# Attention and two feed-forward blocks on one core: where the reciprocals of the softmax sums are written out and spread on SyncE's DMA queue

## The chip, the core and the metric

The kernel runs on one core of one Trainium2 chip. The metric is the device time of one execution in microseconds (us). Before the change it was 748.28 us, the median of 3 runs (746.96 to 752.52).

## The reference

Sixteen heads (2 batches of 8) of 768 tokens and width 64 go through a clustered attention, and the result through two feed-forward blocks. A query sees only the keys whose nearest centroid is its own.

```python
q_assign = np.argmax(np.einsum('bhsd,hcd->bhsc', q_n, c_n), axis=-1)
k_assign = np.argmax(np.einsum('bhsd,hcd->bhsc', k_n, c_n), axis=-1)
mask = q_assign[:, :, :, None] == k_assign[:, :, None, :]
scores = scale * np.matmul(q, k.transpose(0, 1, 3, 2))
scores = np.where(mask, scores, -1000000000.0)
attn = np.exp(scores - max); attn = attn / (sum(attn) + 1e-09)
x = attn @ v                      # then, as (1536 tokens, 512):
x = ((x @ w1) * (x @ w2) @ w3) @ w_out      # as written: h = a * b @ w3
out = (h * clip(h + 3, 0, 6) / 6) @ moe2_w_out,  h = x @ moe2_w_in
```

## The kernel before

The program has three stretches. Up to about 66 us weights are folded (w_out with w3) and the first heads are made ready. From there to about 300 us it does the attention, and after that the two feed-forward blocks with 7-product and 3-product schemes on pieces of 128 x 384. The change touches the attention alone.

**Slots and units.** A slot is one tile of 128 queries of one head against all 768 keys; there are 96 (`SLOTS`). Two heads make a pair of 12 slots, and the slots of a pair are ordered so that 3 tiles of the even head come first, then 3 of the odd head (unit 2p), and then the other 3 and 3 (unit 2p+1). A unit is 6 slots; there are 16. So even head n is first used in slot 6n and odd head n in slot 6n-3.

**One slot.** TensorE makes the scores of slot s+2 (`score`, L1338 and L1340) into one of two PSUM tiles, and can do so only when the exponentials of slot s have left it. VectorE takes the row maximum (`row_max`, L1057), ScalarE the exponential with its row sums (L750). TensorE then transposes the probabilities (L1350), ScalarE and VectorE copy them to `probs_t` (L839, L1117), and TensorE multiplies by V a unit later (`p_times_v`, L1364). Once in a unit TensorE also computes the cluster logits of a coming head (L1308), their columns (L1317) and the one-hot rows (L1325). In iteration s of its loop TensorE issues the scores of slot s+2 first. All engines run through the same iterations, each in its own order.

**The sums.** In the iteration that opens unit u+1 (s = 6u+6) VectorE does, in this order: the row maximum of slot s+2, the reciprocals of unit u's sums (`reciprocals(u)`, L1062 and L1064, which raises the semaphore `s_recip`), and then `x_normed(u-1)` (L1070), which multiplies the attention output of the unit before by its reciprocals. That needs the reciprocals spread over the partitions in `recip_all`. The row maximum of the next slot stands behind it.

**The spreading** goes over DRAM, on SP's queue. `spread_recips(u)` (from L486) waits for `s_recip`, writes the 768 reciprocals to `recip_rows` (L489), waits until they have landed (`s_rrow`), and reads them back twice with a broadcast into `recip_all` (L493, two DMAs, `s_rall`).

**SP's queue.** SP issues its DMAs in the order of the program text, and a wait stops all that follows. For each head n from 2 on:

- `load_ops(n)` (L453): 4 DMAs that copy the split operands of head n to one of three `qk_ops` buffers. It waits until the scores of the head that had the buffer, n-3, are all made: slot 6n-10 for odd n, 6n-13 for even n.
- `load_raw(n+2)` (L465): one DMA, q and k of a later head from DRAM.
- `load_mask(n)` (L459): 6 DMAs that copy the one-hot rows under the operands, after ScalarE has copied them out of PSUM (L742).
- `load_v` (L470): 2 DMAs, for odd n from 5 on.
- `spread_recips(n-3)` for n from 3 on.

The last three units are spread behind the loop, and then the weight blocks of the feed-forward stretch follow on the same queue (L421).

Of the kernel before, what the change touches and what calls it, by code (L numbers as in the profile page):

```python
# [16 lines left out]
ST = S // P  # L17
# [32 lines left out]
def last_slot(n):  # L50

    return n // 2 * 2 * ST + ST + n % 2 * 3 + 2
# [24 lines left out]
def ring_bank(use):  # L77
    return RING[use] % len(RING_BANKS)


def ring_turn(use):

    return RING[use] // len(RING_BANKS)
# [129 lines left out]
def program(nc: bass.Bass, qk, v, cent, wo, w3, w12, wio, out):  # L213
    with ExitStack() as ctx:
        def sem(name):
            return ctx.enter_context(nc.semaphore(name))
# [4 lines left out]
        def sb(name, shape, dt=F32, at=None):  # L221
            size = 4
            for n in shape[1:]:
                size *= n
            size += -size % 64
            if at is None:
                at, top[0] = top[0], top[0] + size
            assert at + size <= nc.sbuf_usable_end, (name, at + size)
            return nc.alloc_sbuf_tensor_at(name, shape, dt, offset=at)
# [23 lines left out]
        sums1, recips = sb("sums1", [P, SLOTS]), sb("recips", [P, SLOTS])  # L253
# [51 lines left out]
        recip_rows = nc.dram_tensor("recip_rows", (2, 2 * HALF), F32, kind="Internal").ap()  # L305
# [18 lines left out]
        s_recip, s_rrow, s_rall = sem("recips_ready"), sem("recip_rows_in"), [sem(f"recips_spread{i}") for i in range(2)]  # L324
# [28 lines left out]
        def x_cols(unit):  # L353

            b, tile = divmod(unit // 2, KT)
            at = tile * TOK + b * S + unit % 2 * HALF
            return slice(at, at + HALF)
# [40 lines left out]
        def _(sp):  # L398
# [42 lines left out]
            def load_ops(n):  # L441
                sp.wait_ge(s_split, 2 * n + 2)
                if n == 2:
                    sp.wait_ge(s_up, F1T)
                if n >= 3:
                    sp.wait_ge(s_scores, last_slot(n - 3) + 1)
                ops, split, done = qk_ops[n % 3], qk_split[n % 2], s_opq[n % 3]
                q_hi = split[0:D, 0:1, :].to_broadcast([D, 2, S])
                for first, operands, source in (
                    (0, slice(0, 2), q_hi), (D, slice(0, 1), split[0:D, 1:2, :]),  # L450
                    (0, slice(2, 4), split[D:P, :, :]), (D, slice(2, 3), split[D:P, 0:1, :]),
                ):
                    sp.dma_start(ops[first:first + D, operands, :].bitcast(F32), source.bitcast(F32)).then_inc(done, 16)  # L453

            def load_mask(n):
                sp.wait_ge(s_rel[ring_bank(("hot", n))], ring_turn(("hot", n)) + 1)
                for rows in range(ST):
                    t = rows % SPANS * 2 + rows // SPANS
                    sp.dma_start(qk_ops[n % 3][D:MASK_ROWS, 1:4:2, t * P:(t + 1) * P].bitcast(F32),  # L459
                                 hot_rows[n % 2][rows * C:(rows + 1) * C, :, :].bitcast(F32)).then_inc(s_opm[n % 3], 16)  # L460

            def load_raw(n):
                sp.wait_ge(s_split, 2 * n - 2)
                sp.wait_ge(s_fill[ring_bank(("logits", n - 2))], ring_turn(("logits", n - 2)) + 1)
                sp.dma_start(qk_raw[n % 2][:], qk[n]).then_inc(s_raw[n % 2], 16)  # L465

            def load_v(n):
                if n >= 4:
                    sp.wait_ge(s_pv, n // 2 * 2 - 2)
                sp.dma_start(v_raw[n % 4][:].rearrange("p t d -> p (t d)"), v[n]).then_inc(s_v[n % 4], 16)  # L470
# [12 lines left out]
            load_mask(1)  # L483
            for n in range(4):
                load_v(n)
            def spread_recips(u):  # L486
                sp.wait_ge(s_recip, u + 1)
                rows = recip_rows[u % 2]
                sp.dma_start(rows.rearrange("(k p t) -> p k t", k=2, t=3),  # L489
                             recips[:, u * ST:(u + 1) * ST].rearrange("p (k t) -> p k t", k=2)).then_inc(s_rrow, 16)  # L490
                sp.wait_ge(s_rrow, 16 * (u + 1))
                for k in range(2):
                    sp.dma_start(recip_all[k * D:(k + 1) * D, x_cols(u)], rows[k * HALF:(k + 1) * HALF].partition_broadcast(D)  # L493
                                 ).then_inc(s_rall[u % 2], 16)

            for n in range(2, HEADS):
                load_ops(n)
                if n + 2 < HEADS:
                    load_raw(n + 2)
                load_mask(n)  # L500
                if n % 2 == 1 and n >= 5:
                    load_v(n - 1)
                    load_v(n)
                if n >= 3:
                    spread_recips(n - 3)
            for u in range(UNITS - 3, UNITS):
                spread_recips(u)
            for n in range(GATE0 + 2, BLOCKS):
                load_next(n)
# [1086 lines left out]
```

## Time and profile before

| | us |
|---|---|
| median of 3 runs | 748.28 (746.96 to 752.52) |
| the profiled execution | 747.12 |
| its span, first to last instruction | 745.1 |

| engine | busy us | share of the span |
|---|---|---|
| PE (TensorE matmuls) | 713.6 | 96% |
| DVE (VectorE) | 470.3 | 63% |
| ACT (ScalarE) | 415.7 | 56% |
| POOL (GpSimd) | 444.3 | 60% |

The profile is one execution, recorded by the hardware. PE is busy nearly all the time, so the question for any change is in which stretches it is not, and what it waits for there. The mean TensorE clock granted over the span is 0.995 of full speed. SPq is the DMA-issuing instructions of SyncE: they are not counted as busy time, but the timeline shows how long each takes. In the chain of work that ended last, TensorE has 68%, DMA 9% and SP's queue 8% of the span.

### The profile page before, as it was taken

To read this page: it belongs to the slowest core of one execution; us is meant where nothing else is said; L and a number is where in the kernel's file an instruction comes from. 1 tells how busy PE (TensorE), PEld (TensorE's weight loads), DVE (VectorE), ACT (ScalarE), POOL (GpSimd) and SP (SyncE) were. 2 spreads that over 40 slices of the span, in tenths; PEclk is the share of its full clock that TensorE was granted. 3 is DMA by queue.
4 is the path that set the end of the run, shared out by engine and by line. 5 is a ranking of instruction groups with operands and counts; after the bars stand their busy time and mean duration, and the time that the engine had idled before them with its cause. 6 is when DMAs were issued, how large, how long until landed. Compare 5 with 4: busy or idle time off the path is not lost.

```text
span 745.1 us, 11781 instructions
## 1 busy us (share of the span) xinstructions
PE 713.6 (96%) x4001; PEld 599.5 (80%) x4001; DVE 470.3 (63%) x706; ACT 415.7 (56%) x855; POOL 444.3 (60%) x453
## 2 busy tenths in 40 slices
PE   6998999988999899999999999999999999999998
PEld 4776666655666466799999999999998779998886
DVE  5326666755666567477886778878865435885221
ACT  6225667656666578444455454467754446775333
POOL 4963343434434356599696996968647748762321
PEclk9999999999999999999999999999999999999999
DMA  9555655555555440121000220002211223221212
GB/s 317 151 150 137 145 144 125 137 122 152 135 124 123 102 100 12 68 86 57 29 29 29 85 70 17 29 29 86 79 63 58 70 81 132 73 72 58 70 43 84
DMA packets 41482, 68.48 MB, mean 92 GB/s; under 512 B 10192, under 2 KB 17360, under 8 KB 41424
## 3 DMA queue, kind: packets, MB, share of 16 engines
q1 hardware_dynamic: 39840, 64.85, 30.6%
q10 hardware_dynamic: 1584, 2.88, 1.0%
q8 instruction: 32, 0.52, 0.3%
q14 instruction: 26, 0.21, 0.1%
HBM read 44.07 MB, written 3.19 MB: 63 GB/s over the span
## 4 chain that ended last, share of the span: by engine, by line
PE 68%; DMA 9%; SPq 8%; DVE 5%; ACT 4%; issue 2%; POOL 2%; ACTq 0%; DVEq 0%; POOLq 0%
PE ps L1260 19%; PE ps L1261 19%; PE ps L1262 18%; SPq L459 5%; DMA recip_rows<-recips 4%; PE ps L1364 3%; DMA recip_all<-recip_rows 3%; PE ps L1350 3%; PE ps L1338 3%; PE ps L1340 2%; DMA stage<-in_w 2%; SPq L453 1%; DVE g_lo L1176 1%; ACT probs L750 1%; DVE sum_lo L1078 1%
## 5 line engine op out<-in xcount | busy, mean ns | idle before, releaser
L596 POOL TENSOR_TENSOR b_lo<-stage,b_hi 128x512 fp32r<-128x512 f32 x94 | 111.7, 1190 | 109.8 <-ACT b_hi L822 107.9
L1176 DVE TENSOR_TENSOR g_lo<-gate,g_hi 128x384 fp32r<-128x384 f32 x96 | 79.7, 838 | 69.1 <-ACT g_hi L882 68.9
L1057 DVE TENSOR_REDUCE neg_max<-ps 128x1 f32<-128x768 f32 x96 | 91.5, 953 | 48.8 <-PE ps L1340 48.8
L882 ACT CAST g_hi<-gate 128x384 fp32r<-128x384 f32 x96 | 48.8, 514 | 83.8 <-PE ps L1262 83.7
L750 ACT ACTIVATE probs<-ps,neg_max 128x768 f32<-128x768 f32 x96 | 86.7, 904 | 15.0 <-DVE neg_max L1057 13.4
L1350 PE MATMUL ps<-ident,probs 128*128 128x128 f32 x576 | 79.9, 275 | 0.6 <-ACT probs_t L839 0.6
L1260 PE MATMUL ps<-b_hi,g_hi 128*128 128x512 f32 x192 | 75.0, 390 | 2.1 <-DVE g_lo L1176 2.1
L1364 PE MATMUL ps<-probs_t,v_raw 128*64 128x384 f32 x384 | 76.3, 507 | 0.0
L839 ACT COPY probs_t<-ps 128x512 f32<-128x512 f32 x96 | 54.4, 585 | 38.5 <-PE ps L1350 38.3
L1261 PE MATMUL ps<-b_lo,g_hi 128*128 128x512 f32 x192 | 74.8, 390 | 0.0
L1262 PE MATMUL ps<-b_hi,g_lo 128*128 128x512 f32 x192 | 74.8, 390 | 0.0
L1078 DVE TENSOR_TENSOR sum_lo<-sum_raw,sum_hi 128x768 fp32r<-128x768 f32 x64 | 64.3, 1009 | 14.7 <-ACT sum_hi L798 14.4
L1350 PEld LDWEIGHTS ps<-ident,probs 128*128 128x128 f32 x576 | 67.3, 141 | 5.9 <-ACT probs_t L839 1.1
L1338 PE MATMUL ps<-qk_ops 128*128 128x512 f32 x192 | 58.5, 386 | 13.3 <-ACT probs L750 11.8
L1151 DVE TENSOR_TENSOR part<-part,ps 128x384 f32<-128x384 f32 x96 | 51.7, 548 | 26.8 <-PE ps L1262 23.2
L798 ACT CAST sum_hi<-sum_raw 128x768 fp32r<-128x768 f32 x64 | 39.4, 617 | 48.8 <-POOL sum_raw L611 30.9
L554 POOL TENSOR_TENSOR hot_cols<-hot,best 128x192 f32<-128x192 f32 x16 | 8.2, 513 | 85.4 <-DVE best L1053 85.4
L859 ACT COPY part<-ps 128x384 f32<-128x384 f32 x96 | 45.9, 478 | 21.7 <-PE ps L1262 21.4
L1338 PEld LDWEIGHTS ps<-qk_ops 128*128 128x128 f32 x192 | 29.2, 191 | 33.6 <-ACT probs L750 21.0
L822 ACT CAST b_hi<-stage 128x512 fp32r<-128x512 f32 x94 | 51.7, 550 | 1.9 <-ACT out_sb L902 1.9
L1340 PE MATMUL ps<-qk_ops 80*128 80x512 f32 x192 | 49.8, 340 | 0.0
L562 POOL TENSOR_TENSOR x_lo<-x_raw,x_hi 128x384 fp32r<-128x384 f32 x15 | 15.0, 1000 | 55.8 <-ACT x_hi L755 55.8
(119 smaller groups left out, 1871.3 us busy)
## 6 DMA issues: line engine op xcount, KB each, us to landing
stage<-in_wio SPq DMA_DIRECT2D x64, 256.0 KB, 2.5
stage<-in_w SPq DMA_DIRECT2D x48, 256.0 KB, 3.1
qk_ops<-qk_split SPq DMA_DIRECT2D x32, 384.0 KB, 5.1
qk_raw<-in_qk SPq DMA_DIRECT2D x16, 384.0 KB, 5.4
qk_ops<-qk_split SPq DMA_DIRECT2D x32, 192.0 KB, 4.8
v_raw<-in_v SPq DMA_DIRECT2D x16, 192.0 KB, 2.6
recip_all<-recip_rows SPq DMA_DIRECT2D x32, 96.0 KB, 2.9
out<-out_sb ACTq DMA_DIRECT2D x11, 256.0 KB, 2.1
```

The source lines that it names most:

```text
L596: nc.gpsimd.tensor_tensor(b_lo[n % 2][:, cols], stage[n % 2][:, cols], b_hi[n % 2][:, cols].bitcast(F32), ALU.subtract).then_inc(s_lo[half ...
L750: nc.scalar.activation(probs[g % PROBS][:], scores[g % 2], ACT.Exp, bias=neg_max[:, g:g + 1], scale=1.0, accum_out=sums[:, g:g + 1]).then_ ...
L1057: nc.vector.tensor_reduce(neg_max[:, g:g + 1], scores[g % 2], AX.X, ALU.max, negate=True).then_inc(s_max, 1)
L1078: nc.vector.tensor_tensor(sum_lo[g % 2][:, cols], sum_raw[:, cols], sum_hi[g % 2][:, cols].bitcast(F32), ALU.subtract).then_inc(s_sum_lo, 1)
L1176: nc.vector.tensor_tensor(g_lo[i][:], hidden(q, c, f)[0][:], g_hi[i][:].bitcast(F32), ALU.subtract).then_inc(s_glo, 1)
L1260: nc.tensor.matmul(psum, w_hi, m_hi, start=start, stop=False, skip_group_check=read_between)
L1261: nc.tensor.matmul(psum, w_hi, m_lo, start=False, stop=False, skip_group_check=read_between)
L1262: return nc.tensor.matmul(psum, w_lo, m_hi, start=False, stop=stop, skip_group_check=read_between)
L1338: nc.tensor.matmul(tile[:, cols], ops[:, 0, q], ops[:, 2, cols], start=True, stop=False)
L1340: mm = nc.tensor.matmul(tile[:, cols], ops[0:MASK_ROWS, 1, q], ops[0:MASK_ROWS, 3, cols], start=False, stop=True)
L1350: mm = nc.tensor.transpose(bank[:, c * P:(c + 1) * P], probs[s % PROBS][:, (j - ST * i) * P:(j - ST * i + 1) * P], ident[:])
L1364: mm = nc.tensor.matmul(ps[side * D:(side + 1) * D, PV_BANKS[unit % 2], 0:HALF].rearrange("p (a b) -> p a b", a=3), v_raw[(unit // 2 * 2 + ...
```

## The change

`spread_recips` is divided in two. `store_recips(u)` waits for the reciprocals and writes them out; it now stands directly behind `load_ops`, ahead of `load_raw` and `load_mask`. `spread_recips(u)` waits until they have landed and reads them back; it now stands behind `load_mask`, and ahead of the two `load_v`. Behind the loop, for the last three units, the two parts follow each other as before. No transfer is added or left out, and no other engine's program differs.

```diff
-            def spread_recips(u):
-                sp.wait_ge(s_recip, u + 1)
-                rows = recip_rows[u % 2]
-                sp.dma_start(rows.rearrange("(k p t) -> p k t", k=2, t=3),
-                             recips[:, u * ST:(u + 1) * ST].rearrange("p (k t) -> p k t", k=2)).then_inc(s_rrow, 16)
-                sp.wait_ge(s_rrow, 16 * (u + 1))
+            def store_recips(u):
+                sp.wait_ge(s_recip, u + 1)
+                sp.dma_start(recip_rows[u % 2].rearrange("(k p t) -> p k t", k=2, t=3),
+                             recips[:, u * ST:(u + 1) * ST].rearrange("p (k t) -> p k t", k=2)).then_inc(s_rrow, 16)
+
+            def spread_recips(u):
+                sp.wait_ge(s_rrow, 16 * (u + 1))
+                rows = recip_rows[u % 2]
                 for k in range(2):
                     sp.dma_start(recip_all[...], rows[...].partition_broadcast(D)).then_inc(s_rall[u % 2], 16)

             for n in range(2, HEADS):
                 load_ops(n)
+                if n >= 3:
+                    store_recips(n - 3)
                 if n + 2 < HEADS:
                     load_raw(n + 2)
                 load_mask(n)
+                if n >= 3:
+                    spread_recips(n - 3)
                 if n % 2 == 1 and n >= 5:
                     load_v(n - 1)
                     load_v(n)
-                if n >= 3:
-                    spread_recips(n - 3)
             for u in range(UNITS - 3, UNITS):
+                store_recips(u)
                 spread_recips(u)
```

On SP's queue, for an odd head (n = 5, whose one-hot rows are in `hot_rows_74`), from the last operand copy on; rows with - stand there before the change, rows with + after it:

```order
 L453 DMA qk_ops_59<-qk_split_63 64x768
+L488 DMA recip_rows<-recips 128x2x3 [waits recips_ready]
 L465 DMA qk_raw_61<-in_qk 128x768 [waits ring_filled0,qk_split]
 L459 DMA qk_ops_59<-hot_rows_74 16x2x128 [waits ring_released0]
 L459 DMA qk_ops_59<-hot_rows_74 16x2x128 x5
+L495 DMA recip_all<-recip_rows 64x384 [waits recip_rows_in]
+L495 DMA recip_all<-recip_rows 64x384
 L470 DMA v_raw_69<-in_v 128x384 [waits pv_filled]
 L470 DMA v_raw_70<-in_v 128x384 [waits pv_filled]
-L489 DMA recip_rows<-recips 128x2x3 [waits recips_ready]
-L493 DMA recip_all<-recip_rows 64x384 [waits recip_rows_in]
-L493 DMA recip_all<-recip_rows 64x384
```

The writing-out has moved ahead of 7 DMAs and, like the spreading, ahead of the two loads of V, which now come last.

On SP's queue, for the even head before it (n = 4), up to the first operand copy of head 5:

```order
 L453 DMA qk_ops_58<-qk_split_62 64x768
+L488 DMA recip_rows<-recips 128x2x3 [waits recips_ready]
 L465 DMA qk_raw_60<-in_qk 128x768 [waits ring_filled0,qk_split]
 L459 DMA qk_ops_58<-hot_rows_73 16x2x128 [waits ring_released0]
 L459 DMA qk_ops_58<-hot_rows_73 16x2x128 x5
-L489 DMA recip_rows<-recips 128x2x3 [waits recips_ready]
-L493 DMA recip_all<-recip_rows 64x384 [waits recip_rows_in]
-L493 DMA recip_all<-recip_rows 64x384
+L495 DMA recip_all<-recip_rows 64x384 [waits recip_rows_in]
+L495 DMA recip_all<-recip_rows 64x384
 L453 DMA qk_ops_59<-qk_split_63 64x2x768 [waits scores_filled,qk_split]
```

Only the writing-out has moved; the wait for the reciprocals (`recips_ready`) now stands ahead of the raw load and the one-hot rows.

## Rows read from the trace of the kernel before

**Rows 1.** Windows by start and end: length, busy time, PE clock, DMA share.

```profile
core 0: us, PE busy (x) PEld busy (x) DVE busy (x) ACT busy (x) POOL busy (x), PEclk, DMA share, GB/s
124.19:138.50 14.31, 14.31 (x96) 9.58 (x95) 9.76 (x17) 10.06 (x22) 6.44 (x9) 1.00 0.60 129
138.50:156.53 18.03, 15.87 (x97) 10.71 (x95) 9.99 (x17) 10.57 (x23) 7.45 (x10) 0.91 0.58 150
247.00:251.40 4.40, 4.40 (x21) 2.00 (x21) 1.65 (x2) 2.41 (x5) 3.71 (x5) 0.63 0.55 139
309.00:745.00 436.00, 428.99 (x2282) 403.01 (x2281) 287.28 (x391) 230.00 (x476) 298.94 (x277) 1.00 0.18 62
```

**Rows 2.** Waits of PE, 60 to 310 us: total us, times, longest.

```profile
PE ps L1338 <- ACT probs L750: 11.8, 9, 3.5
```

**Rows 3.** Timeline of PE: start, length, instruction, idle before and its releaser.

```profile
79.20 0.63 PE L1308 MATMUL ps<-qk_raw,cent_t 128*32 128x256 f32 x6
...
131.09 0.52 PE L1340 MATMUL ps<-qk_ops 80*128 80x512 f32 x2
...
148.11 0.61 PE L1338 MATMUL ps<-qk_ops 128*128 128x512 f32 x2
...
152.68 1.01 PE L1338 MATMUL ps<-qk_ops 128*128 128x512 f32 x2 [2.16 <-ACT probs L750]
...
250.37 1.08 PE L1308 MATMUL ps<-qk_raw,cent_t 128*32 128x256 f32 x6
```

**Rows 4.** Timeline of DVE around two turns of the reciprocals.

```profile
133.59 0.19 DVE L1064 RECIPROCAL recips<-sums 128x6 f32<-128x6 f32 x1
...
147.89 0.19 DVE L1064 RECIPROCAL recips<-sums 128x6 f32<-128x6 f32 x1
150.53 0.66 DVE L1070 TENSOR_TENSOR x_raw<-ps,recip_all 128x384 f32<-128x384 f32 x1 [2.44 <-DMA recip_all<-recip_rows]
```

**Rows 5.** Waits of DVE, 66 to 278 us: total us, times, longest.

```profile
DVE x_raw L1070 <- DMA recip_all<-recip_rows: 14.1, 9, 3.8
```

**Rows 6.** Timeline of SP's queue for head 7: start, length, DMAs.

```profile
131.68 3.79 SPq L453 DMA_DIRECT2D qk_ops<-qk_split  x4
135.57 1.75 SPq L465 DMA_DIRECT2D qk_raw<-in_qk  x1
137.36 4.48 SPq L459 DMA_DIRECT2D qk_ops<-hot_rows  x6
141.88 1.05 SPq L470 DMA_DIRECT2D v_raw<-in_v  x2
142.98 0.43 SPq L489 DMA_DIRECT2D recip_rows<-recips  x1
145.80 1.13 SPq L493 DMA_DIRECT2D recip_all<-recip_rows  x2
```

**Rows 7.** Chain of work that ended last, pieces from 140 to 158 us.

```profile
146.34 4.10 DMA recip_all<-recip_rows
...
151.64 0.99 ACT probs L750 x2
```

**Rows 8.** Waits of SP's queue, 66 to 273 us.

```profile
SPq L493 <- DMA recip_rows<-recips: 36.7, 13, 5.5
SPq L446 <- PE ps L1340: 8.7, 5, 2.9
```

**Rows 9.** Line 489, all 16 writings-out: from issue to landing.

```profile
DMA to landing us min/median/max: 2.2/3.1/5.9
```

**Rows 10.** Line 493, all 32 spreadings: from issue to landing.

```profile
DMA to landing us min/median/max: 2.5/2.9/4.1
```

**Rows 11.** Line 453, operand copies: from issue to landing.

```profile
DMA to landing us min/median/max: 3.8/4.7/6.1
```

**Rows 12.** Line 459, one-hot rows: from issue to landing.

```profile
DMA to landing us min/median/max: 1.8/2.3/4.1
```

## The prediction

> **What bounds the kernel now.** I read the windows first, then the waits of TensorE, then the chain of work back from one such wait, and last the timeline of SP's queue against VectorE's. After 309 us the change moves nothing, and TensorE is busy 428.99 of 436.00 us there [rows 1]; all that can be won or lost lies in the attention. There TensorE has a pace of its own. From one set of logits to the next is one unit, and the unit from 124.19 to 138.50 us has no idle time: 14.31 us at full clock. The next one takes 18.03 us with 15.87 busy, at a mean clock of 0.91 [rows 1]. Between the logits at 79.20 and those at 250.37 us lie 11 units in 171.17 us [rows 3]; at 14.31 each they would take 157.41, so 13.8 us are lost there. The waits of TensorE say to whom: nine times, 11.8 us in all, the scores (L1338) wait for an exponential [rows 2].
>
> What holds the exponential is seen in the unit of 138.50 to 156.53. VectorE ends the reciprocals of a unit at 148.08 (147.89 + 0.19) and could do x_normed then; it starts it at 150.53, having waited 2.44 us for the spread reciprocals [rows 4]. The row maximum queued behind it is late, so are the two exponentials at 151.64 [rows 7], and the scores at 152.68 come after 2.16 us idle [rows 3]. So the wait on VectorE costs TensorE all but 0.3 us. VectorE has nine such waits, 14.1 us [rows 5]; less 0.3 each that is 11.4, and TensorE's nine are 11.8 [rows 2]: the same ones. And SP is what makes the reciprocals late: it stands 36.7 us in 13 waits between writing out and spreading, and for scores, its wait when it is ahead of TensorE, only 5 times, 8.7 us [rows 8].
>
> **What the change does to an odd head.** Head 7 is a clean case, since SP is on time for it. Its trigger is the end of the scores at 131.61 (131.09 + 0.52) [rows 3], and the copies start at 131.68 [rows 6]. VectorE's turn at 148.08 [rows 4] is 16.5 us behind the trigger: one unit of 14.31 plus 2.2. Before, the spreading lands at 150.44 (146.34 + 4.10) [rows 7], 18.8 us behind the trigger, so 2.4 late even with SP on time. After the change, by the same rows [rows 6]:
>
> - spreading starts at 145.80. Taken away: the loads of V ahead of it (142.98 - 141.88 = 1.10) and all from the start of the writing-out to the spreading (145.80 - 142.98 = 2.82). Added ahead: the issue of the writing-out, up to 0.6 us with its gap (0.43 here; I take the larger). So 142.5.
> - if it lands as slowly as it did here (0.54 to the second issue, then 4.10), that is 147.1, 1.0 us before the turn. With the median 2.9 [rows 10] it is 145.9, 2.1 us before.
>
> So the wait goes to nothing with a slack of 1.0 to 2.1 us. The bounds of that landing are the 2.5 and 4.1 of the same transfers [rows 10]; it now follows the one-hot rows directly, and I take 3.5, nearer to the upper end, because nothing drains the queue ahead of it any more. The slack is then 1.5 us.
>
> **The writing-out now lies behind the operand copies.** It is issued 3.9 us after the first of them, and the spreading asks for it at 142.5, about 6.9 us behind its issue (135.6). Before it took 2.2 to 5.9 us to land [rows 9]. The cost of its new place is not in the trace. Lower bound: as before, 3.1, wholly hidden under the raw load and the six one-hot issues (1.75 + 4.48 us [rows 6]). Upper bound: it can only start to count when the last copy, issued about 1 us earlier, has landed, up to 6.1 us after its issue [rows 11], and then takes its worst 5.9: 5.1 + 5.9 = 11.0 us, 4.1 too late. With the medians it is 3.7 + 3.1 = 6.8 us, which just fits. I take 0 for it, as it fits and 1.5 us of slack stand behind; the upper bound makes a rival below.
>
> The Trainium skill (DMA: Bandwidth & Descriptors, section "Queues, rings and completion order") speaks against the change here. It says that descriptors are consumed in ring order, and that the increment of the semaphore is a strongly ordered write, which lands only after that engine's earlier writes. By it the 3 KB would wait for some 1.1 MB of copies ahead of them, so the 3.7 us would always be paid and the landing would be at least 3.7 + 2.2 = 5.9 us. No row here shows a small transfer directly behind these copies, so it is open whether the trace agrees; even by the rule the sum stays as it is, since 5.9 and 6.8 both lie within the 6.9.
>
> **The wait for the reciprocals now stands ahead of raw load and one-hot rows.** For an odd head the reciprocals of unit n-3 are ready at 133.78 (133.59 + 0.19) [rows 4], 2.2 us behind the trigger, and the copies keep SP until 135.5 [rows 6]: no wait. For the even head 8 behind it: SP starts its copies when head 7 is done, 142.5 + 1.13 + 1.10 + gaps = 144.8, and has issued them at 148.7; the reciprocals are ready at 148.08: no wait. Then writing-out, raw load and one-hot rows (0.6 + 1.8 + 4.0) and the spreading (1.2 to issue) take it to 156.3, and the spreading lands at 158.6 to 159.9. The turn is at 148.08 + 14.31 = 162.4. The next trigger, 2 x 14.31 behind the last one, is at 160.2, so SP has 3.9 us to spare in each pair and comes on time to the next odd head. Before, the same sum is longer by two waits of 2.2 us or more each (2.82 less the issue), so SP has nothing to spare: that is why heads further on are late by more than 2.4 us (up to 3.8 [rows 5]).
>
> **The other moves.** The one-hot rows of head 7 are issued 0.6 us later, the last at 141.9, landing by 144.2 to 146.0 [rows 12]. TensorE's first scores of head 7 are those at 148.11 [rows 3]: at least 2.1 us of cover. The loads of V move behind the spreading by 1.2 us; they are for products two units on. Both cost nothing. For the last three units the order is as before.
>
> **The sum.** Idle time: 11.8 us [rows 2]. Half clock: after the two longest waits TensorE is granted less for a while. The unit of 18.03 us has 3.72 more than 14.31, of which 2.16 idle, so 1.56 from the clock; the stretch from 247.00 lasts 4.40 us at a mean of 0.63 [rows 1], 4.40 x 0.37 = 1.6. Together 15.0 us. Against the units: 13.8 for the eleven, and the rest falls behind 250.37. I keep back 0.6 us for a few landings at the upper end: 14.4 us. Of the profiled execution's 747.1 us that leaves 732.7; the median of the runs is 1.2 us higher and gives 733.9. I forecast 733.5 us.
>
> **The rivals.**
> - The writing-out lands late (**rival A**, 0.12). If the last copy must land and HBM be slow as well, the spreading waits up to 4.1 us. Beyond 1.5 us of slack and TensorE's 0.3 it costs 2.3 us in each of the seven odd heads (3 to 15) whose turns were late: 16 us, nothing is left of the gain. In the middle, with landings of 9.9 us (3.0 late), it is 1.2 x 7 = 8 us, so 741 us. For it: nothing shows the new place. Against: the medians fit.
> - Another wait takes the place (**rival B**, 0.07). A unit after a stalled one may run at 14.31 us only because the stall gave the others time. Then the pace would be that of SP or VectorE, and the time 744 to 749 us. Against: in the clean unit VectorE is busy 9.76 and ScalarE 10.06 of 14.31 us, and GpSimd 6.44 [rows 1]; SP's issues sum to some 12 us of 14.31.
> - The one-hot rows of the odd heads come late (**rival C**, slower, 0.03). They now follow one more transfer and land among a queue that never drains. It decides from a landing of 6.2 us (148.11 - 141.9), against 4.1 at most now [rows 12]. To be slower by 1% they would have to cost 15.0 + 7.5 us over seven heads, 3.2 us each beyond that point, landing after 9.4 us: 756 us.
>
> **How the numbers follow.** My forecast, a gain of 12 to 15.5 us, has 0.78; the rivals have 0.12, 0.07 and 0.03. More than 1% (7.5 us) is what a measurement can tell from none. Faster: 0.78 and half of A, 0.84. Same: the rest of A and B, 0.13. Slower: C, 0.03. Lower end of the range: the fastest run, 746.96, less 15.0, less 1.5 for what the runs scatter: 730.5. Upper end: the middle of A, 741.
>
> **What would show it.** Right: no wait for the spread reciprocals on VectorE ahead of L1070 before the last units, and TensorE's 11.8 us of L1338 waiting for L750 gone; 14.3 us from logits to logits in all units; SP waiting for scores ahead of every odd head's copies, several us each. Wrong: SP still waiting for the written-out rows ahead of the spreading by more than 1.5 us in odd heads (A), VectorE still waiting in x_normed, or TensorE waiting for a DMA of `qk_ops` (C). It would also be wrong if the units ran at 14.31 us and the feed-forward stretch grew in return.

## The result, and the profile of the changed kernel

| | before | changed |
|---|---|---|
| median of 4 runs, us | 749.94 (746.96 to 752.52) | 731.43 (730.17 to 731.85) |
| the profiled execution, us | 747.12 | 731.85 |
| its span, us | 745.1 | 729.8 |
| mean TensorE clock over the span | 0.995 | 1.000 |

The ratio of the runs is 0.9752, with a 95% interval of 0.9708 to 0.9796: 18.5 us faster. Between the two profiled executions it is 15.3 us, because that of the kernel before was one of its faster ones.

The first view is the page's list of the chain that ended last, by engine. Before it had DMA and SP's queue with 17% together.

```profile
PE 89%; DVE 5%; ACT 3%; POOL 2%; issue 1%; DMA 1%; ACTq 0%; SPq 0%; POOLq 0%
```

DMA now has 1% and SP's queue none. The windows and the timeline of TensorE show the attention. (The lines of this kernel are 5 higher than before from `spread_recips` on: L1313 was L1308, L1330 was L1325, L1343 was L1338, L1345 was L1340, L1069 was L1064, L1075 was L1070. L488 writes out and L495 spreads.)

```profile
77.64:234.94 157.30, 157.30 (x1037) 105.39 (x1035) 107.24 (x177) 110.50 (x232) 66.57 (x87) 1.00 0.74 145
```

```profile
77.64 0.63 PE L1313 MATMUL ps<-qk_raw,cent_t 128*32 128x256 f32 x6
...
144.27 0.42 PE L1330 MATMUL ps<-ident,hot_cols 128*96 128x128 f32 x2
144.44 0.60 PE L1343 MATMUL ps<-qk_ops 128*128 128x512 f32 x2
...
234.94 0.63 PE L1313 MATMUL ps<-qk_raw,cent_t 128*32 128x256 f32 x6
```

The same eleven units that took 171.17 us in [rows 3] take 157.30 us, and TensorE is busy in all of them: 14.30 us each, the pace of the one clean unit of [rows 1]. The group of [rows 2] is gone from its waits. What is left between 60 and 295 us is small, and stood there before too (its two longest items are shown):

```profile
PE ps L1330 <- POOL hot_cols L563: 2.2, 2, 1.4
PE ps L1355 <- ACT probs_t L844: 0.6, 2, 0.3
```

The waits of SP's queue between 66 and 262 us answer to [rows 8]:

```profile
SPq L446 <- PE ps L1345: 25.4, 7, 4.2
SPq L488 <- DVE recips L1069: 3.2, 1, 3.2
SPq L495 <- DMA recip_rows<-recips: 1.9, 1, 1.9
```

The 36.7 us in 13 waits for written-out rows are now 1.9 us in one, and that one and the 3.2 us for the reciprocals are behind the loop, where nothing was moved. In their place SP waits 25.4 us in 7 times for TensorE's scores, 3.6 us ahead of each odd head: it is no longer what is late. Head 7 again, on SP's queue and on VectorE, as in [rows 4, 6]:

```profile
128.02 3.75 SPq L453 DMA_DIRECT2D qk_ops<-qk_split  x4
131.81 1.80 SPq L488 DMA_DIRECT2D recip_rows<-recips  x1
133.71 0.71 SPq L465 DMA_DIRECT2D qk_raw<-in_qk  x1
134.46 4.34 SPq L459 DMA_DIRECT2D qk_ops<-hot_rows  x6
138.85 1.23 SPq L495 DMA_DIRECT2D recip_all<-recip_rows  x2
140.13 1.06 SPq L470 DMA_DIRECT2D v_raw<-in_v  x2
```

```profile
144.23 0.19 DVE L1069 RECIPROCAL recips<-sums 128x6 f32<-128x6 f32 x1
144.38 0.67 DVE L1075 TENSOR_TENSOR x_raw<-ps,recip_all 128x384 f32<-128x384 f32 x1
```

The spreading starts 10.8 us behind the first copy (138.85 - 128.02), where it was 14.1 (145.80 - 131.68). With 0.64 us to the second of the two and the median landing of 3.0 it has landed at 142.5 (in this head it took 2.7, so 142.2); VectorE's turn comes at 144.4 and it goes straight on. The slack by the median is 1.9 us. By their own landings it is 1.4 to 2.3 us over the seven odd heads, 2.2 in head 7.

**Where 15.3 us of the span went.** The attention from the first of those logits to the first product of the feed-forward stretch took 221.5 us and now takes 206.0: 15.4 us less. The rest is two differences that cancel. The stretch ahead of it was 1.6 us shorter and the feed-forward stretch 1.7 us longer (444.4 against 446.1 us). Both are taken up with the experiments.

### The profile page after: what moved, and what is told of

The parts are those of the page before. It is cut to its first block, busy times and chain, and to the rows that moved or that the text cites. A ratio compares the mean times of both kernels' runs of the same rounds, so it can differ in the third digit from the quotient of the medians.

```text
span 729.8 us, 11781 instructions
## 1 busy us (share of the span) xinstructions
PE 711.2 (97%) x4001; PEld 598.6 (82%) x4001; DVE 468.1 (64%) x706; ACT 415.8 (57%) x855; POOL 442.1 (61%) x453
## 4 chain that ended last, share of the span: by engine, by line
PE 89%; DVE 5%; ACT 3%; POOL 2%; issue 1%; DMA 1%; ACTq 0%; SPq 0%; POOLq 0%
PE ps L1265 20%; PE ps L1266 19%; PE ps L1267 19%; PE ps L1369 10%; PE ps L1355 8%; PE ps L1343 5%; PE ps L1345 4%; DVE g_lo L1181 2%; PE ps L1313 1%; DVE sum_lo L1083 1%; PE ps L1330 1%; DMA stage<-in_w 1%; PE ps L1322 1%; ACT out_sb L907 1%; POOL b_lo L601 1%
## 5 line engine op out<-in xcount | busy, mean ns | idle before, releaser
L1083 DVE TENSOR_TENSOR sum_lo<-sum_raw,sum_hi 128x768 fp32r<-128x768 f32 x64 | 64.3, 1008 | 14.4 <-ACT sum_hi L803 14.1
L1343 PE MATMUL ps<-qk_ops 128*128 128x512 f32 x192 | 58.2, 384 | 0.0
L1345 PE MATMUL ps<-qk_ops 80*128 80x512 f32 x192 | 49.5, 339 | 0.0
L1175 DVE SCALAR_TENSOR_TENSOR gate<-gate,part 128x384 f32<-128x384 f32 x48 | 38.5, 801 | 15.1 <-ACT gate L873 15.1
L873 ACT ACTIVATE gate<-part,three 128x384 f32<-128x384 f32 x48 | 29.8, 620 | 27.7 <-DVE part L1156 27.7
```

What stands on the lines that cost most here:

```text
L1083: nc.vector.tensor_tensor(sum_lo[g % 2][:, cols], sum_raw[:, cols], sum_hi[g % 2][:, cols].bitcast(F32), ALU.subtract).then_inc(s_sum_lo, 1)
L1343: nc.tensor.matmul(tile[:, cols], ops[:, 0, q], ops[:, 2, cols], start=True, stop=False)
L1345: mm = nc.tensor.matmul(tile[:, cols], ops[0:MASK_ROWS, 1, q], ops[0:MASK_ROWS, 3, cols], start=False, stop=True)
```

## The experiments

All are compared with the kernel before on the same chip. In the four comparisons its medians were 749.9, 744.1, 748.9 and 748.5 us. The changed kernel was run in the first and, as a control, in the last of them, at 731.4 and 732.2 us; the other kernels are set against these two times, some of them from another comparison.

| experiment | median us | ratio to before, 95% |
|---|---|---|
| no reciprocals over DRAM | 730.76 | 0.9796 to 0.9855 |
| divided in odd heads only | 731.06 | 0.9797 to 0.9854 |
| divided in even heads only | 746.30 | 0.9973 to 1.0040 |
| divided, V ahead of the spreading | 731.23 | 0.9803 to 0.9868 |
| in one piece, ahead of V | 743.88 | 0.9907 to 0.9962 |
| spreading directly behind writing-out | 742.85 | 0.9889 to 0.9952 |
| raw load first, then writing-out | 730.09 | 0.9734 to 0.9808 |
| 2, 4, 6 small DMAs ahead of the spreading | 730.78, 734.42, 741.47 | 0.9739 to 0.9810, 0.9786 to 0.9845, 0.9882 to 0.9940 |
| 6 small DMAs behind the spreading | 731.55 | 0.9750 to 0.9806 |
| the changed kernel again | 732.20 | 0.9763 to 0.9826 |

### Is it the wait for the reciprocals, and all of it?

The kernel before, without the calls of `spread_recips`, and with a constant tile in place of `recip_all`, so that the normalisation is left out:

```diff
-                if n >= 3:
-                    spread_recips(n - 3)
...
-                dve.wait_ge(s_rall[unit % 2], 32 * (unit // 2 + 1))
...
-                                        recip_all[:, cols].rearrange("p (q t) -> p t q", t=3), ALU.mult)
+                                        cent_t[:].rearrange("p a b -> p (a b)")[:, 0:HALF].rearrange("p (q t) -> p t q", t=3), ALU.mult)
```

> The kernel before without any reciprocal DMA: nothing is written out or spread, and x_normed multiplies by a constant tile instead and waits for no transfer (the normalisation is left out, and the output is another). My theory: all that the change won is the wait of x_normed, so this runs as the changed kernel does, about 731 us, with no wait of TensorE on L750 in the attention. Rival theory (the DMAs themselves or SP's busy queue cost something beyond that wait): clearly less than 731, 725 or below. Rival theory (the gain came from where the raw loads or one-hot rows stand): stays near 748.

It ran in 730.76 us. With the whole round trip gone, it is no faster than the changed kernel within the runs' spread (730.6 to 732.4 against 730.2 to 733.7). So the round trip costs nothing any more, and the wait of `x_normed` was all there was to win. The DMAs as such, their bytes and their time on SP's queue, cost nothing that these runs can tell.

### Which heads?

The two parts divided for odd heads alone, and for even heads alone (`par` is 1 or 0; for the other heads all stays behind V):

```diff
                 load_ops(n)
+                if n >= 3 and n % 2 == par:
+                    store_recips(n - 3)
...
                 load_mask(n)
+                if n >= 3 and n % 2 == par:
+                    spread_recips(n - 3)
...
+                if n >= 3 and n % 2 != par:
+                    store_recips(n - 3)
+                    spread_recips(n - 3)
```

> The two parts are divided only for odd heads; for even heads writing-out, wait and spreading stay together at the end. My theory: the odd heads have the short deadline (16.5 us from trigger to turn), and SP's queue takes 12.7 us for an odd head and about 14.4 for an even one, 27.1 of the 28.6 us of a pair, so it is still on time at each trigger: 731 to 734 us, nearly the whole gain. Rival theory (what counts is the time that SP's queue is relieved of, whichever head): half the gain, about 740 us.

> The two parts are divided only for even heads; for odd heads all stands as before, V ahead. My theory: SP is now on time at each trigger, but the spreading for an odd head still lands 17 to 18.8 us behind it with the turn at 16.5, so x_normed waits 1 to 2.4 us in each of seven turns: 738 to 746 us, the smaller part of the gain. Rival theory (SP's time, whichever head): half the gain, about 740 us, with SP late at the triggers.

Odd heads alone gave 731.06 us, the whole gain. Even heads alone gave 746.3 us, none of it (before: 744.1 in the same comparison), 0.3 us above what my theory allowed. The trace of the second shows why. Its waits of DVE up to 265 us, of PE up to 300 and of SP's queue up to 265:

```profile
DVE x_raw L1078 <- DMA recip_all<-recip_rows: 11.0, 6, 2.6
```

```profile
PE ps L1346 <- ACT probs L758: 11.2, 7, 2.3
```

```profile
SPq L446 <- PE ps L1348: 19.7, 7, 6.4
```

SP is on time there, it waits for scores 7 times, and still the spreading of an odd head comes late. With head 15, whose wait of 1.9 us lies behind 265, `x_normed` waits 13.0 us in exactly the seven odd heads. In the kernel before the nine waits were those seven, 12.4 us, and two even heads, 4 and 10, 1.7 us; only the latter are gone. So the backlog of SP's queue, which I had given a part in the waits, was not what decided: the chain of a single odd head from its trigger was too long, and that is the same whether SP had spare time before it or not. The rival that only SP's total counts would have split the gain in two halves; it falls.

### Which of the two moves: the division, or going ahead of V?

Against the changed kernel, the first leaves V ahead:

```diff
                 load_mask(n)
-                if n >= 3:
-                    spread_recips(n - 3)
                 if n % 2 == 1 and n >= 5:
                     load_v(n - 1)
                     load_v(n)
+                if n >= 3:
+                    spread_recips(n - 3)
```

and the second leaves the two parts together:

```diff
                 load_ops(n)
-                if n >= 3:
-                    store_recips(n - 3)
...
                 load_mask(n)
                 if n >= 3:
+                    store_recips(n - 3)
                     spread_recips(n - 3)
```

> As the changed kernel, but the loads of V stay ahead of the spreading. My theory: the spreading comes 1.1 us later, of 1.9 us of slack in the changed kernel's trace (lands at 142.5, turn at 144.4): no loss, 731 to 732 us, no wait in x_normed or one or two short ones. Rival theory (the V loads' new place made a part of the gain): 735 us or more.

> The kernel before with one edit: the spreading in one piece, moved ahead of the V loads. My theory: an odd head's spreading lands 1.1 us earlier, 16.6 to 17.7 us behind the trigger against a turn at 16.5, and SP's queue still has no time to spare, so the waits of x_normed shrink by about 1 us each and remain: a third to a half of the gain, 738 to 743 us. Rival theory (the V loads' place made the gain): near 731 us.

With V ahead and the parts divided it ran in 731.23 us, with no wait in `x_normed` up to 278 us: the division is enough by itself. It only just is: in head 13 the second spreading lands at 230.6 us and is used at 230.7. In one piece ahead of V it ran in 743.88 us, 5.0 us faster than before in its comparison, with 11.7 us in 9 waits of `x_normed` up to 278 us, where [rows 5] has 14.1 in 9. That is about a quarter of the gain, a little less than I expected. The 1.1 us taken off in each odd head did not reach VectorE in full: 5.3 of the 11.7 us are now waits in four even heads (4, 6, 8 and 10), where the kernel before had 1.7 in two. The edit leaves the bare waits on SP's queue (31.4 us in 12), and SP is ahead of TensorE only 3 times, so here its backlog is the likely cause of the waits in even heads. The two moves do not add up: once there is slack, the second is worth nothing.

### How much slack is there?

Small DMAs that nobody reads (16 rows of 512 bytes from a constant tile to DRAM) in each odd head, k = 2, 4, 6 of them ahead of the spreading, or 6 behind it (SP also waits once for the constant tile ahead of the loop, and for the added DMAs at the end):

```diff
                 load_mask(n)
+                if n >= 3 and n % 2 == 1:
+                    for i in range(k):
+                        sp.dma_start(pad[n * k + i], ident[0:C, :]).then_inc(s_pad, 16)
                 if n >= 3:
                     spread_recips(n - 3)
```

> As the changed kernel, with two small DMAs (16 rows of 512 bytes, read by nobody) issued ahead of the spreading in each odd head, 1.2 us. My theory: the slack there is about 1.9 us, so nothing is lost: 731 to 732 us. Rival theory (no slack, the change only just got there): 1 us in each of seven heads, 738 us.

> As the changed kernel, with four small DMAs (16 rows of 512 bytes, read by nobody) issued ahead of the spreading in each odd head, 2.4 us. My theory (the spreading has about 1.9 us of slack there, and TensorE covers another 0.3): 0 to 0.5 us are lost in each of seven heads, 731 to 735 us, with short waits in x_normed. Rival theory (the slack is the 3.9 us that SP has to spare in a pair): 731 us, no wait.

> The same with six small DMAs ahead of the spreading, 3.6 us. My theory: 1.7 us late, 1.4 of them for TensorE, in each of seven heads, 738 to 744 us. Rival theory (only SP's total matters, 3.9 us to spare): 731 us.

> The same six small DMAs in each odd head, but behind the spreading and ahead of the V loads. Same traffic and same time on SP's queue, but not ahead of the reciprocals. My theory: SP has 3.9 us to spare in a pair and these take 3.6, so it is just on time: 731 to 734 us. Rival theory (it is the traffic or SP's total that costs): as with six ahead.

They took 0.5 us each to issue, a little less than the 0.6 I had reckoned. Two ran in 730.78 us; four in 734.42, six in 741.47; six behind the spreading in 731.55. Waits of DVE (up to 265 us) and PE with four, then with six:

```profile
DVE x_raw L1082 <- DMA recip_all<-recip_rows: 3.8, 5, 1.0
```

```profile
PE ps L1350 <- ACT probs L762: 2.6, 5, 0.7
```

```profile
DVE x_raw L1082 <- DMA recip_all<-recip_rows: 9.1, 6, 2.0
```

```profile
PE ps L1350 <- ACT probs L762: 8.2, 6, 1.7
```

With four, the spreading of head 7 starts 13.1 us behind the first copy, 2.2 later than in the changed kernel, and `x_normed` waits 0.5 us there and 0.8 on average in five heads. With six it starts 14.2 us behind it, 3.4 later, and `x_normed` waits 2.0 us there and 1.4 on average in seven heads (the seventh, 0.9 us, lies behind 265). So the slack of head 7 comes out at 1.7 and 1.4 us, a little less than the 1.9 to 2.2 in the trace of the changed kernel, and TensorE covers another 0.2 of each wait. The control with the same DMAs behind the spreading settles the rival: the same traffic and the same load on SP's queue cost nothing there that the runs can tell, since SP has some 3.6 us to spare in a pair and these take 2.9. Its trace has two short waits in `x_normed`, 1.4 us in all, in the even heads 8 and 12, so that spare time is nearly used up.

### What if the wait is taken at once?

```diff
                 load_ops(n)
                 if n >= 3:
                     store_recips(n - 3)
+                    spread_recips(n - 3)
                 load_raw(n + 2)
                 load_mask(n)
-                if n >= 3:
-                    spread_recips(n - 3)
```

> As the changed kernel, but the spreading follows the writing-out directly, ahead of the raw load and the one-hot rows. My theory: the wait is bare again, and longer, about 5 us, as the writing-out lies behind the operand copies; the one-hot rows of odd heads land 17.3 to 19.5 us behind the trigger and TensorE needs them at 16.5, and SP needs some 32 us for a pair against 28.6: TensorE waits for the one-hot rows, 745 to 758 us. Rival theory (all that counts is that the reciprocals are spread early): 731 us.

It ran in 742.85 us: 0.8% faster than before, but most of the gain is gone, and the loss was smaller than I expected: the bare wait is 3.0 us on average (38.8 in 13) instead of some 5. The reciprocals are spread earliest of all, and `x_normed` waits nowhere. The waits of PE between 62 and 300 us, SP's queue for head 7, and PE at the first scores of head 7:

```profile
PE ps L1342 <- issue: 10.8, 6, 3.3
```

```profile
136.49 1.79 SPq L488 DMA_DIRECT2D recip_rows<-recips  x1
141.85 1.11 SPq L495 DMA_DIRECT2D recip_all<-recip_rows  x2
143.06 0.53 SPq L465 DMA_DIRECT2D qk_raw<-in_qk  x1
143.63 3.86 SPq L459 DMA_DIRECT2D qk_ops<-hot_rows  x6
```

```profile
148.83 0.58 PE L1342 MATMUL ps<-qk_ops 128*128 128x512 f32 x2 [2.53 <-issue]
```

SP stands 3.6 us bare between writing out and spreading (141.85 - 136.49 - 1.79), and the one-hot rows behind it are issued up to 147.5. The profile names no releaser for TensorE's wait; the last one-hot DMA starts at 146.9 and with 1.8 us of landing is there at 148.7, just before the scores start. This is the mechanism of my rival C, made on purpose: had the change been put one step further ahead, the wait would only have moved from VectorE to TensorE.

### Does the writing-out take long to issue?

The raw load and the writing-out change places.

```diff
                 load_ops(n)
-                if n >= 3:
-                    store_recips(n - 3)
                 if n + 2 < HEADS:
                     load_raw(n + 2)
+                if n >= 3:
+                    store_recips(n - 3)
                 load_mask(n)
```

> As the changed kernel, but the writing-out stands behind the raw load and ahead of the one-hot rows. In the changed kernel its issue takes 1.7 us and the raw load's 0.7, where they took 0.5 and 1.6 before. My theory: the long issue belongs to the place right behind the four copies, so here the raw load takes about 1.6 and the writing-out 0.5 us; it has 1.2 us less cover and lands after some 4.5 to 5 us, so that the spreading waits 0 to 0.5 us: 731 to 732.5 us. Rival theory (the writing-out is slow to issue by its own 256 small pieces): 1.7 us there too.

It ran in 730.09 us, as fast as the changed kernel within the runs. SP's queue for head 7:

```profile
132.06 1.75 SPq L465 DMA_DIRECT2D qk_raw<-in_qk  x1
133.85 0.68 SPq L488 DMA_DIRECT2D recip_rows<-recips  x1
134.58 4.66 SPq L459 DMA_DIRECT2D qk_ops<-hot_rows  x6
```

The long issue belongs to the place: in this head whoever comes first behind the four copies takes 1.75 to 1.8 us, and the next one 0.7.

### Chance, or the change?

> The changed kernel once more, as a control: 731 us. In its first profile the stretch before 78 us was 1.6 us shorter than in the kernel before and the feed-forward stretch 1.7 us longer, with the same instructions; if both are chance they come out elsewhere here, if the change makes them they come again.

The control took 732.2 us (profiled span 729.5). The stretch ahead of the attention ended early again, the first logits at 77.4 us. They stand between 77.5 and 78.2 us also in the other kernels, but at 81.0 in the one with six DMAs ahead. TensorE starts its first scores at 53.17 us in the kernel before, after a wait of 1.53 for the first one-hot rows, at 53.46 with six DMAs ahead, and at 51.4 in the control. So the difference of the kernel before is there by then, and about half of that of the other. The first instruction that the change moves is issued at 75.6 us, so the change did not make it. How often the kernel before starts late can't be said from its one profile. The feed-forward stretch took 446.1 us in the control, as in the first profile of the changed kernel, so by my own test chance is not shown for it. In the others it took 444.3 to 444.5 (the kernel before, no reciprocals, odd heads only, raw first, at once, six ahead), 445.1 to 445.2 (five of them), or 446.1 (four ahead as well). The steps are 0.9 us, and they come in kernels of either kind: with and without the division, with and without TensorE's waits. Whether the changed kernel always has the longest of the three times can't be said from two profiles; the last section shows one step.

## Why the prediction was right

The forecast was 733.5 us, the range 730.5 to 741.0; it measured 731.43.

- **The bound** was TensorE's waits for the exponential behind `x_normed`. Right: 14.30 us in every unit, and with the round trip taken away altogether it is no faster.
- **The sum** had 15.0 us, less 0.6 kept back. The attention became 15.4 us shorter between the two profiled executions. The 0.6 was not needed: there is no wait of `x_normed` at all before the last units. The 18.5 us between the medians hold 3 us more, because the kernel before runs at 741 to 754 us from one execution to the next and the reference of the sum was one of its fast ones; the prediction spoke only of the 1.2 us to the median then known. In the control's comparison the difference of the medians is 16.3 us.
- **The odd head.** Spreading was to start 10.8 us behind the first copy, and starts 10.8 behind it. Two terms in that were wrong and cancelled: the writing-out takes 1.80 us to issue, not 0.6, and the raw load behind it 0.71 instead of 1.75. The slack was to be 1.0 to 2.1 us, and is 1.9 to 2.2 in the trace of this head and 1.4 to 1.7 by the added DMAs.
- **The landing of the writing-out** was taken at 6.8 us by the medians, with 6.9 at hand. It has a median of 4.9 and a maximum of 6.8, so rival A did not come; but in head 7 it landed at 138.6, only 0.2 us before it was asked for. The rule of the Trainium skill (DMA: Bandwidth & Descriptors, "Queues, rings and completion order"), that a later increment lands behind the earlier writes of the same DMA engine, agrees with the trace here: the last copy of head 7 is issued at 130.8 and lands 7.6 us later, at 138.4, and the 3 KB issued at 131.8 land 0.2 us behind it. In all 13 heads they land behind the last copy, by 0.2 to 1.8 us. What the prediction worked out from the rule, 3.7 + 2.2 = 5.9 us at least, does not hold: eleven of the 13 land sooner, after 4.6 us at the least, so the writing-out does not take its full 2.2 us again behind the last copy.

```profile
L453 SPq DMA_DIRECT2D qk_ops<-qk_split x1: 1003/1003/1003, 130.8 to 130.8; - x1
...
DMA to landing us min/median/max: 7.6/7.6/7.6
```

```profile
L488 SPq DMA_DIRECT2D recip_rows<-recips x1: 1805/1805/1805, 131.8 to 131.8; - x1
...
DMA to landing us min/median/max: 6.8/6.8/6.8
```

- **SP's spare time** was to be 3.9 us in a pair; it waits 3.6 for each odd head's trigger. Right in size. What I made of it was not: that the missing spare time "is why heads further on are late". Nor are they late by more than 2.4 us as a rule: of the nine waits one is 3.8 us, and the others are 2.4 or less. Even heads alone gave SP its spare time and won nothing. (The sum for the even head took 4.0 us for the issue of the six one-hot rows, where [rows 6] has 4.48; that accounts for most of the difference to 3.6.)
- **The nine waits** are explained in the prediction for odd heads alone. Two of them, 1.7 us, stood in even heads (4 and 10); they went too.
- **The waits for the reciprocals** ahead of the raw load cost nothing before the last units, as said.
- **The one-hot rows** were to land after 4.1 us at most. They take up to 6.0 now (median 4.0 instead of the 2.3 of [rows 12]): the raw load is issued 0.7 us ahead of them instead of 1.8. It is the first ones that take so long. In head 7 the last is issued at 138.2, lands at 141.7 and is needed at 144.4; the least cover of an odd head is 2.0 us, in heads 11 and 13. So rival C did not come, though the landing that it was priced with, 4.1 at most, was exceeded. With the raw load first they have their 2.3 us back, and the time is the same; that is the order with more cover.
- **The clock** held 1.00 through the attention, so the 3.2 us counted for it came.
- **The feed-forward stretch** grew by 1.7 us, which the prediction had named as a sign of being wrong. It is a ninth of the gain, and the kernel without the round trip or with odd heads divided has the gain and the shorter stretch (444.4 us). That it does not show in the total is chance: the stretch ahead of the attention was 1.6 us shorter in the same profile, and the sum had neither.

## What to carry to other kernels

A wait for a round trip on a queue that issues for others is paid twice, by what stands behind it and by whoever needs its result; put the first half ahead of work that must be issued anyway and the second half behind it, and check three things in the trace: that the inputs of the first half are ready at its new place, how long it takes to land behind what it now follows, and when the work in between is needed. Measure the slack with harmless transfers ahead of the second half. Look for the one deadline that is missed before you relieve the queue as a whole: the parts divided in the odd heads brought everything here, those in the even heads nothing.

## What was not expected of the hardware

**An issue that takes 1.7 us by its place.** On SP's queue the first DMA behind the four operand copies takes 1.1 to 2.1 us to issue, mostly 1.6 to 1.8, be it a 384 KB load or 3 KB, and nearly all after it 0.4 to 0.8. A profile read before such a move gives the issue time of the place, not of the transfer.

**The scatter of the kernel before.** It ran in 741.5 to 754.3 us, and the three kernels in which most of TensorE's waits stayed (even heads only, in one piece ahead of V, spreading at once) spread over 7.8, 4.8 and 5.1 us in 10 executions each. The changed kernel stayed within 730.2 to 733.7 in 8. It looks as if the bare waits made the scatter, but the kernel with six DMAs ahead waits too and spread over 2.5 us in 4 executions, so this is not shown. What is on record is the clock: in the comparison with the most executions of the kernel before, the five fastest (745.0 to 747.0 us) had a mean granted clock of 0.997 to 1.000, and the three slowest (752.4 to 754.3 us) 0.991. By an estimate 0.009 of 746 us is 6.7 us, most of the difference. In the profile before, the clock is low right behind two of the nine waits ([rows 1] has 0.63 from 247.00 on), and the kernels whose waits are gone or at most 1.7 us long have 0.998 to 1.000 in every execution. So what a wait costs beyond its own length differs from one execution to the next. The order is less clear in the kernel with even heads only: its 742.0 and its 749.8 us both have 0.995.

**A race of 0.03 us that is worth 0.9.** In the feed-forward stretch VectorE and GpSimd each start an operation with two inputs in SBUF at almost the same time. In the kernel before VectorE starts first, at 374.64 against 374.67:

```profile
374.64 0.56 DVE L1176 TENSOR_TENSOR g_lo<-gate,g_hi 128x384 fp32r<-128x384 f32 x1 [1.09 <-ACT g_hi L882]
```

```profile
374.67 1.40 POOL L653 TENSOR_TENSOR mix<-mix,mix 128x384 f32<-128x384 f32 x1
```

In the changed kernel GpSimd does, at 357.65 against 357.67:

```profile
357.67 1.42 DVE L1181 TENSOR_TENSOR g_lo<-gate,g_hi 128x384 fp32r<-128x384 f32 x1 [1.12 <-ACT g_hi L887]
```

```profile
357.65 1.02 POOL L658 TENSOR_TENSOR mix<-mix,mix 128x384 f32<-128x384 f32 x1
```

Whoever comes second waits, and VectorE's 0.86 us go into the chain that ended last. The Trainium skill (SBUF — State Buffer, section "SBUF: two separate sides") says that the two engines share a pair of ports as an exclusive lock, which the first to start holds for its whole instruction, and that a VectorE operation with two SBUF inputs takes part in it against a GpSimd operation that reads SBUF. The trace agrees: VectorE takes 1.42 us as the second and 0.56 as the first, GpSimd 1.40 and 1.02. It is a likely source of the 0.9 us steps of this stretch, but only this one place is shown; that all of them are such races is not.
